# Twelve weight tiles of a split-precision gated MLP, each started at its own offset within 128 bytes

## The chip, the cores and the metric

The kernel runs on one NeuronCore of one Trainium2 chip. The metric is device time in microseconds of one execution. The time before is the median of 3 runs; one further execution was profiled.

## What is computed

The reference takes a transposed-channel attention over q, k, v (6016 rows of 256 channels) and sends its result through two gated feed-forward layers of width 1536:

```python
qn = q / (norm(q, axis=rows) + 1e-6);  kn = the same of k
a = softmax(kn^T @ qn / tau);  x = v @ a
def moe(x):                              # layer 1
    xn = x / sqrt(mean(x*x) + 1e-6) * rms_g
    g = xn @ w1_gate
    return (g * sigmoid(g) * (xn @ w1_val)) @ w1_out
def moe2(x):                             # layer 2
    return (sigmoid(x @ w2_gate) * (x @ w2_val)) @ w2_out
out = moe2(moe(x))
```

## The kernel before

All matrix products of the layers are made in the matmul format fp32r from operands that are split in a high and a low part: a product is hi x hi + hi x lo + lo x hi, three matmuls of 128x128 weights and up to 512 moving columns that add up in one PSUM bank (`three`, L682 to L684, and in `down`, L813 to L815). Activations are held transposed, channels on partitions, in blocks of 512 tokens: eleven full blocks (the trace's 128x512 matmuls) and a last one of 384.

For each block and layer TensorE walks over twelve slices j of 128 hidden channels. `up` makes gate and value of a slice (two banks, six matmuls each, weights from `w_hi_g`, `w_lo_g`, `w_hi_v`, `w_lo_v`, moving operands `xs` or `x2`, high and low). `down`, two slices behind, multiplies the gated slice (`h_hi`, `h_lo`) by the output weights (`w_hi_o`, `w_lo_o`) into two banks, three matmuls each. That makes 18 large matmuls per slice. The order of work is written out by hand: `plan` interleaves layer 2 of block b with layer 1 of block b+2, and every engine walks the same plan with semaphores between them. ScalarE makes the sigmoid and rounds to the high parts (L405, L411), VectorE multiplies and makes the low parts (L613, L617, L622). Into layer 2's slices `next_x` puts the next block of the attention product (`make_x`), its row sums of squares (`sum_squares`, L708, short fp32 matmuls with one moving column) and the spreading of the row factors (`spread_rms`, L717).

There are six weights: gate, value and out of layer 1 (g1, v1, o1) and of layer 2 (g2, v2, o2). Each has a tile `w_hi` and a tile `w_lo`, so twelve in all, of 3072 floats per partition (12288 bytes, 96 times 128). The raw fp32 weights (`w_raw`) are loaded by DMA on SP's queue to where `w_lo` will stand and are split in place: ScalarE rounds (L335, for o2 L331), VectorE (L463, layer 1) or GpSimd (L319, L315, layer 2) subtracts. The SBUF allocator puts the tiles one after another; a tile of 24 floats called `align` stands between the small tiles and the matmuls' activations. All twelve weight tiles and all moving tiles (`xs`, `x2`, `h_hi`, `h_lo`) begin at a multiple of 128 bytes.

Ahead of the layers TensorE multiplies q and k over 47 row tiles in plain fp32 (L751, two matmuls in the trace for each of the program), and then, while the softmax is made by the other engines, it runs products that nobody reads, to stay busy: `keep_warm` (L728). Fifty of them take `w_hi_g` of layer 1 both as weights and as moving operand. They differ in form. The first 23 are four plain ones, four with 126 weight columns, four with 96, four whose weight columns are 16 bytes apart, four whose 256 moving columns are 8 bytes apart, and three whose weights begin 4 bytes further on. Then follow six with 256 moving columns (before `sum_squares(0)`), four whose weights begin 8 bytes on and six whose weights begin 256 bytes on (before `spread_rms(0)`), and eleven more, six of which change between two PSUM banks and five of which take one weight column 128 times.

Of the kernel before, what the change touches and what calls it, by code (L numbers as in the profile page):

```python
# [23 lines left out]
F32 = mybir.dt.float32  # L24
F32R = mybir.dt.float32r
# [4 lines left out]
P = 128  # L30
SQ = 32
# [6 lines left out]

def build(nc, q, k, v, tau, rms_g, w1_gate, w1_val, w1_out, w2_gate, w2_val, w2_out, out):
    _, N, C = q.shape  # L40
    F = w1_gate.shape[1]
    CC = C // P
    J = F // P
    JG = J // GROUPS
# [48 lines left out]
    with ExitStack() as ctx:  # L93
        def sb(name, shape, dt=F32):
            return ctx.enter_context(nc.sbuf_tensor(name, shape, dt))
# [5 lines left out]
        W = ("g1", "v1", "o1", "g2", "v2", "o2")  # L101
        shape = {w: [P, J, C] if w[0] == "o" else [P, CC, F] for w in W}

        w_hi = {w: sb(f"w_hi_{w}", shape[w], F32R) for w in W[:3]}
        with ExitStack() as early:
            w_raw = {w: early.enter_context(nc.sbuf_tensor(f"w_raw_{w}", shape[w], F32)) for w in W}
        w_lo = {w: sb(f"w_lo_{w}", shape[w], F32R) for w in W[:3]}
        with ExitStack() as early:  # L110
            qk = early.enter_context(nc.sbuf_tensor("qk", [P, QK_SLOTS, 2, QK_TILES * C], F32))
            sq_qk = early.enter_context(nc.sbuf_tensor("sq_qk", [P, 2, 2, QK_TILES * C], F32))
            sum_sq = early.enter_context(nc.sbuf_tensor("sum_sq", [P, 2, 2 * C], F32))
        w_lo.update({w: sb(f"w_lo_{w}", shape[w], F32R) for w in W[3:]})
        w_hi.update({w: sb(f"w_hi_{w}", shape[w], F32R) for w in W[3:]})

        ident = sb("ident", [P, P])
        ones = sb("ones", [P, P])
# [21 lines left out]
        ps = ctx.enter_context(nc.psum_tensor("ps", [P, 8, BLOCK], F32))  # L140
        GATE, VALUE = (0, 2), (1, 3)
        Y, X = (4, 5), (6, 7)
# [530 lines left out]
        def _(pe):  # L673
# [13 lines left out]
            def make_x(b, vt):  # L687
                w = width(b)
                pe.wait_ge(vt_lo_done, b * 2 + 2)
                for d in range(CC):  # L690
                    three(ps[:, X[d], 0:w],
                          [(a_hi[:, c, d * P:(d + 1) * P], a_lo[:, c, d * P:(d + 1) * P], vt[0][:, c, 0:w],
                            vt[1][:, c, 0:w]) for c in range(CC)]).then_inc(x_made, 1)

            def sum_squares(b):
                nt = width(b) // P


                first = isinstance(b, int) and b == 0
                chunks_left = CC if first else 1  # L700
                if first:
                    pe.wait_ge(x_squared, CC)
                    pe.wait_ge(xg_done, 1)
                else:
                    pe.wait_ge(squares_added, b)
                for n in range(nt):
                    for c in range(chunks_left):
                        mm = nc.tensor.matmul(ps[:, X[0], n:n + 1], sq[:, c, n * P:(n + 1) * P], ones[:, 0:1],  # L708
                                              start=(c == 0), stop=(c == chunks_left - 1))
                mm.then_inc(ms_made, 1)  # L710

            def spread_rms(b, diag):

                w = width(b)
                for part in range(2):
                    pe.wait_ge(diag_done, b * 2 + part + 1)
                    mm = nc.tensor.matmul(ps[:, X[1], 0:w], ones_r[:, :], diag[part][:, 0, 0:w],  # L717
                                          start=(part == 0), stop=(part == 1))
                mm.then_inc(rinv_spread, 1)

            def keep_warm(n, weights, cols=None, bank=Y[1]):

                cols = w_hi["g1"][:, 0, 0:JG * P] if cols is None else cols
                dst = ps[:, bank, 0:JG * P]
                if cols.shape[1] < JG * P:
                    dst = ps[:, bank, 0:cols.shape[1]]
                for _ in range(n):
                    nc.tensor.matmul(dst[0:weights.shape[-1], :], weights, cols, start=True, stop=True)  # L728

            def column_norms():  # L730

# [12 lines left out]
            for i, slot, t0, n in chunks:  # L744
# [4 lines left out]
                for t in range(n):  # L749
                    for c in range(CC):  # L750
                        mm = nc.tensor.matmul(ps[:, RAW[c], 0:C], alternate(qk[:, slot, 1, t * C:(t + 1) * C], c),  # L751
                                              qk[:, slot, 0, t * C:(t + 1) * C],
                                              start=(t0 + t == 0), stop=(t0 + t == TILES - 1))
# [2 lines left out]
            nc.tensor.matmul(ps[:, SPREAD, 0:C], ones[:, :], q_diag.rearrange("p c m -> p (c m)"),  # L756
                             start=True, stop=True).then_inc(q_spread, 1)
            pe.wait_ge(w_hi_done, 1)
            any_w = w_hi["g1"]
            keep_warm(4, any_w[:, 0, 0:P])  # L760
            keep_warm(4, any_w[:, 0, 0:P - 2])
            keep_warm(4, any_w[:, 0, 0:96])
            keep_warm(4, any_w[:, 0, 0:JG * P:JG])
            keep_warm(4, any_w[:, 0, 0:P], any_w[:, 0, 0:JG * P:2])
            keep_warm(3, any_w[:, 0, 1:P + 1])
            pe.wait_ge(a_lo_done, CC)
            make_x(0, xs)
            keep_warm(6, any_w[:, 0, 0:P], any_w[:, 0, 0:JG * P // 2])
            sum_squares(0)
            pe.wait_ge(ones_r_done, 1)  # L770
            keep_warm(4, any_w[:, 0, 2:P + 2])
            keep_warm(6, any_w[:, 0, 64:P + 64])
            spread_rms(0, xs)
            for _ in range(3):
                keep_warm(1, any_w[:, 0, 0:P], bank=Y[0])
                keep_warm(1, any_w[:, 0, 0:P], bank=Y[1])
            keep_warm(5, any_w[:, 0, 0:1].broadcast_to([P, P]))

            def up(layer, b, j, x, parts_of_x):

# [122 lines left out]
```

## Time and profile before

| | |
|---|---|
| median of 3 runs | 1273.71 us (1273.67 to 1273.84) |
| the profiled execution | 1273.06 us, span of its instructions 1271.3 us |
| TensorE matmul busy | 1259.9 us, 99% of the span, 5710 matmuls |
| weight loads busy | 1059.0 us (83%) |
| VectorE, ScalarE, GpSimd busy | 659.7, 454.7 and 41.4 us |
| DMA X

A matmul's end is modelled and matmuls overlap in the array: one is printed as 0.39 us long although the next begins 0.23 us after it. What a matmul costs is the distance between two starts. The weight loads (PEld) run beside the matmul before.

### The profile page before, as it was taken

To read this page: it belongs to the slowest core of one execution; us is meant where nothing else is said; L and a number is where in the kernel's file an instruction comes from. 1 tells how busy PE (TensorE), PEld (TensorE's weight loads), DVE (VectorE), ACT (ScalarE), POOL (GpSimd) and SP (SyncE) were. 2 spreads that over 40 slices of the span, in tenths; PEclk is the share of its full clock that TensorE was granted. 3 is DMA by queue.
4 is the path that set the end of the run, shared out by engine and by line. 5 is a ranking of instruction groups with operands and counts; after the bars stand their busy time and mean duration, and the time that the engine had idled before them with its cause. 6 is when DMAs were issued, how large, how long until landed. Compare 5 with 4: busy or idle time off the path is not lost.

```text
span 1271.3 us, 15532 instructions
## 1 busy us (share of the span) xinstructions
PE 1259.9 (99%) x5710; PEld 1059.0 (83%) x5710; DVE 659.7 (52%) x1014; ACT 454.7 (36%) x737; POOL 41.4 (3%) x35
## 2 busy tenths in 40 slices
PE   8999999999999999999999999999999999999998
PEld 7878888888888888888888888888888888889888
DVE  6776654544554554554454455455455455446343
ACT  5453633333333333333333333333333333333332
POOL 0000600000000000000000000000000000000000
PEclk9999999999999999999999999999999999999999
DMA  9920000100100100010010010010010001000000
GB/s 345 305 87 1 1 1 1 34 0 0 33 0 0 33 0 0 8 25 0 0 33 0 0 33 0 0 33 0 0 29 4 0 0 29 1 1 18 1 17 13
DMA packets 60569, 34.43 MB, mean 27 GB/s; under 512 B 50816, under 2 KB 54144, under 8 KB 60544
## 3 DMA queue, kind: packets, MB, share of 16 engines
q1 hardware_dynamic: 60544, 34.09, 9.3%
q8 instruction: 16, 0.26, 0.1%
q14 instruction: 9, 0.07, 0.0%
HBM read 27.92 MB, written 6.16 MB: 27 GB/s over the span
## 4 chain that ended last, share of the span: by engine, by line
PE 98%; DMA 0%; DVE 0%; SPq 0%; POOL 0%; issue 0%; DVEq 0%
PE ps L682 21%; PE ps L684 21%; PE ps L683 21%; PE ps L813 10%; PE ps L815 10%; PE ps L814 10%; PE ps L751 3%; PE ps L708 1%; PE ps L728 1%; DMA qk<-in_k 0%; PE ps L717 0%; SPq L257 0%; POOL small L303 0%; PE ps L737 0%; DVE w_lo_v L463 0%
## 5 line engine op out<-in xcount | busy, mean ns | idle before, releaser
L617 DVE TENSOR_TENSOR h<-ps,h 128x512 f32<-128x512 f32 (+1 forms) x288 | 196.0, 680 | 304.9 <-PE ps L684 291.4
L411 ACT ACTIVATE h_hi<-h 128x512 fp32r<-128x512 f32 (+1 forms) x288 | 179.4, 623 | 397.8 <-DVE h L617 396.2
L405 ACT ACTIVATE h<-ps 128x512 f32<-128x512 f32 (+1 forms) x288 | 169.6, 589 | 376.6 <-PE ps L684 376.5
L622 DVE TENSOR_TENSOR h_lo<-h,h_hi 128x512 fp32r<-128x512 f32 (+1 forms) x288 | 199.3, 692 | 130.7 <-ACT h_hi L411 127.0
L815 PE MATMUL ps<-h_hi,w_lo_o 128*128 128x512 f32 (+1 forms) x576 | 221.6, 385 | 0.0
L813 PE MATMUL ps<-h_hi,w_hi_o 128*128 128x512 f32 (+1 forms) x576 | 221.5, 385 | 0.0
L814 PE MATMUL ps<-h_lo,w_hi_o 128*128 128x512 f32 (+1 forms) x576 | 221.5, 385 | 0.0
L613 DVE TENSOR_TENSOR h<-ps,h 128x512 f32<-128x512 f32 (+1 forms) x144 | 97.9, 680 | 148.6 <-ACT h L405 148.6
L815 PEld LDWEIGHTS ps<-h_hi,w_lo_o 128*128 128x128 f32 x576 | 108.1, 188 | 20.7
L813 PEld LDWEIGHTS ps<-h_hi,w_hi_o 128*128 128x128 f32 x576 | 108.1, 188 | 20.6
L814 PEld LDWEIGHTS ps<-h_lo,w_hi_o 128*128 128x128 f32 x576 | 108.1, 188 | 20.5
L682 PE MATMUL ps<-xs_hi,w_hi_g 128*128 128x512 f32 (+1 forms) x312 | 119.0, 381 | 0.6 <-DVE w_lo_v L463 0.6
L684 PE MATMUL ps<-xs_hi,w_lo_g 128*128 128x512 f32 (+1 forms) x312 | 118.8, 381 | 0.0
L683 PE MATMUL ps<-xs_lo,w_hi_g 128*128 128x512 f32 (+1 forms) x312 | 118.8, 381 | 0.0
L684 PE MATMUL ps<-xs_hi,w_lo_v 128*128 128x512 f32 (+1 forms) x312 | 118.7, 381 | 0.0
L682 PE MATMUL ps<-xs_hi,w_hi_v 128*128 128x512 f32 (+1 forms) x312 | 118.7, 381 | 0.0
L683 PE MATMUL ps<-xs_lo,w_hi_v 128*128 128x512 f32 (+1 forms) x312 | 118.7, 381 | 0.0
L682 PE MATMUL ps<-x_hi,w_hi_g 128*128 128x512 f32 x264 | 103.7, 393 | 0.0
L684 PE MATMUL ps<-x_hi,w_lo_g 128*128 128x512 f32 x264 | 102.9, 390 | 0.0
L682 PE MATMUL ps<-x_hi,w_hi_v 128*128 128x512 f32 x264 | 102.8, 389 | 0.0
L683 PE MATMUL ps<-x_lo,w_hi_g 128*128 128x512 f32 x264 | 102.8, 389 | 0.0
L684 PE MATMUL ps<-x_hi,w_lo_v 128*128 128x512 f32 x264 | 102.8, 389 | 0.0
(113 smaller groups left out, 1324.1 us busy)
## 6 DMA issues: line engine op xcount, KB each, us to landing
v_in<-in_v SPq DMA_DIRECT2D x44, 128.0 KB, 3.0
out<-out_sb SPq DMA_DIRECT2D x44, 128.0 KB, 2.4
qk<-in_q SPq DMA_DIRECT2D x10, 512.0 KB, 7.6
qk<-in_k SPq DMA_DIRECT2D x10, 512.0 KB, 9.1
w_raw_g<-in_moe_w_gate SPq DMA_DIRECT2D x6, 512.0 KB, 7.6
w_raw_v<-in_moe_w_val SPq DMA_DIRECT2D x6, 512.0 KB, 8.2
w_raw_o<-in_moe_w_out SPq DMA_DIRECT2D x6, 512.0 KB, 8.8
qk<-in_q SPq DMA_DIRECT2D x3, 256.0 KB, 3.3
```

The lines of the kernel that those rows point to most:

```text
L405: nc.scalar.activation(h[:, slot, 0:w], ps[:, GATE[slot], 0:w], ACT.Sigmoid).then_inc(sig_done, 1)
L411: nc.scalar.activation(h_hi[:, part, 0:w], h[:, slot, 0:w], ACT.Copy).then_inc(hi_done, 1)
L613: nc.vector.tensor_tensor(h[:, slot, 0:w], ps[:, GATE[slot], 0:w], h[:, slot, 0:w], ALU.mult).then_inc(gated_done, 1)
L617: nc.vector.tensor_tensor(h[:, slot, 0:w], ps[:, VALUE[slot], 0:w], h[:, slot, 0:w], ALU.mult).then_inc(h_done, 1)
L622: nc.vector.tensor_tensor(h_lo[:, part, 0:w], h[:, slot, 0:w], h_hi[:, part, 0:w].bitcast(F32), ALU.subtract).then_inc(lo_done, 1)
L682: nc.tensor.matmul(dst, s_hi, m_hi, start=(n == 0), stop=False)
L683: nc.tensor.matmul(dst, s_hi, m_lo, start=False, stop=False)
L684: mm = nc.tensor.matmul(dst, s_lo, m_hi, start=False, stop=(n == last))
L751: mm = nc.tensor.matmul(ps[:, RAW[c], 0:C], alternate(qk[:, slot, 1, t * C:(t + 1) * C], c), qk[:, slot, 0, t * C:(t + 1) * C], start=(t0 ...
L813: nc.tensor.matmul(dst, hi, h_hi[:, part, 0:w], start=(j == 0), stop=False)
L814: nc.tensor.matmul(dst, hi, h_lo[:, part, 0:w], start=False, stop=False)
L815: mm = nc.tensor.matmul(dst, lo, h_hi[:, part, 0:w], start=False, stop=(j == J - 1))
```

## The change

Every weight tile is allocated 32 floats longer (12416 bytes, 97 times 128), so that the tiles still begin at multiples of 128 bytes, and the 3072 floats that are used begin at an offset of their own in it. In bytes: high parts g1 16, v1 32, o1 48, g2 4, v2 120, o2 96; low parts g1 64, v1 80, o1 112, g2 8, v2 124, o2 0. The raw weights, which share the place of the low parts, have their offsets. The moving tiles still begin at multiples of 128 bytes, each 1536 bytes higher in SBUF. The second part of the change makes all matmuls of `keep_warm` alike: plain weights, 512 moving columns, one bank, 23 + 6 + 10 + 12 of them.

```diff
-        w_hi = {w: sb(f"w_hi_{w}", shape[w], F32R) for w in W[:3]}
+        START_HI = {"g1": 4, "v1": 8, "o1": 12, "g2": 1, "v2": 30, "o2": 24}
+        START_LO = {"g1": 16, "v1": 20, "o1": 28, "g2": 2, "v2": 31, "o2": 0}
+
+        def weight_tile(stack, name, w, dt, start):
+
+            tile = stack.enter_context(nc.sbuf_tensor(name, [P, CC * F + SQ], dt))
+            return tile[:, start:start + CC * F].rearrange("p (a b) -> p a b", a=shape[w][1])
+
+        w_hi = {w: weight_tile(ctx, f"w_hi_{w}", w, F32R, START_HI[w]) for w in W[:3]}
         with ExitStack() as early:
-            w_raw = {w: early.enter_context(nc.sbuf_tensor(f"w_raw_{w}", shape[w], F32)) for w in W}
-        w_lo = {w: sb(f"w_lo_{w}", shape[w], F32R) for w in W[:3]}
+            w_raw = {w: weight_tile(early, f"w_raw_{w}", w, F32, START_LO[w]) for w in W}
+        w_lo = {w: weight_tile(ctx, f"w_lo_{w}", w, F32R, START_LO[w]) for w in W[:3]}
...
-        w_lo.update({w: sb(f"w_lo_{w}", shape[w], F32R) for w in W[3:]})
-        w_hi.update({w: sb(f"w_hi_{w}", shape[w], F32R) for w in W[3:]})
+        w_lo.update({w: weight_tile(ctx, f"w_lo_{w}", w, F32R, START_LO[w]) for w in W[3:]})
+        w_hi.update({w: weight_tile(ctx, f"w_hi_{w}", w, F32R, START_HI[w]) for w in W[3:]})
...
-            keep_warm(4, any_w[:, 0, 0:P])
-            keep_warm(4, any_w[:, 0, 0:P - 2])
-            keep_warm(4, any_w[:, 0, 0:96])
-            keep_warm(4, any_w[:, 0, 0:JG * P:JG])
-            keep_warm(4, any_w[:, 0, 0:P], any_w[:, 0, 0:JG * P:2])
-            keep_warm(3, any_w[:, 0, 1:P + 1])
+            keep_warm(23)
             pe.wait_ge(a_lo_done, CC)
             make_x(0, xs)
-            keep_warm(6, any_w[:, 0, 0:P], any_w[:, 0, 0:JG * P // 2])
+            keep_warm(6)
             sum_squares(0)
             pe.wait_ge(ones_r_done, 1)
-            keep_warm(4, any_w[:, 0, 2:P + 2])
-            keep_warm(6, any_w[:, 0, 64:P + 64])
+            keep_warm(10)
             spread_rms(0, xs)
-            for _ in range(3):
-                keep_warm(1, any_w[:, 0, 0:P], bank=Y[0])
-                keep_warm(1, any_w[:, 0, 0:P], bank=Y[1])
-            keep_warm(5, any_w[:, 0, 0:1].broadcast_to([P, P]))
+            keep_warm(12)
```

No other instruction of any engine is added, removed or moved. On TensorE, from the last matmul of the first `make_x` to the first of the layers, this stood before:

```order
L684 MATMUL ps<-xs_hi,a_lo 128x512
L728 MATMUL ps<-w_hi_g 128x256 x6
L708 MATMUL ps<-ones,scratch 128x1 x8
L728 MATMUL ps<-w_hi_g 128x512 x10
L717 MATMUL ps<-xs_hi,ones_r 128x512
L717 MATMUL ps<-xs_lo,ones_r 128x512
L728 MATMUL ps<-w_hi_g 128x512 x11
L682 MATMUL ps<-xs_hi,w_hi_g 128x512
```

And this stands there now:

```order
L692 MATMUL ps<-xs_hi,a_lo 128x512
L732 MATMUL ps<-w_hi_g 128x512 x6
L716 MATMUL ps<-ones,scratch 128x1 x8
L732 MATMUL ps<-w_hi_g 128x512 x10
L725 MATMUL ps<-xs_hi,ones_r 128x512
L725 MATMUL ps<-xs_lo,ones_r 128x512
L732 MATMUL ps<-w_hi_g 128x512 x12
L690 MATMUL ps<-xs_hi,w_hi_g 128x512
```

Six matmuls ahead of the sums of squares are twice as wide, and one more stands ahead of the layers.

## Rows read from the trace of the kernel before

**Rows 1.** The page: busy time by engine, and the TensorE clock in 40 slices.
```profile
PE 1259.9 (99%) x5710; PEld 1059.0 (83%) x5710; DVE 659.7 (52%) x1014; ACT 454.7 (36%) x737; POOL 41.4 (3%) x35
PEclk9999999999999999999999999999999999999999
```

**Rows 2.** Chain of waits, stretch of one loop turn (start us, us, what).
```profile
497.14 0.79 PE ps L708 x8
...
599.19 0.79 PE ps L708 x8
```

**Rows 3.** Matmuls and loads by line and form (count, busy us, mean ns, idle us).
```profile
L815 PE MATMUL ps<-h_hi,w_lo_o 128*128 128x512 f32 x528 | 205.5, 389 | 0.0
L682 PE MATMUL ps<-x_hi,w_hi_g 128*128 128x512 f32 x264 | 103.7, 393 | 0.0
L683 PE MATMUL ps<-xs_lo,w_hi_v 128*128 128x512 f32 x264 | 102.7, 389 | 0.0
L813 PE MATMUL ps<-h_hi,w_hi_o 128*128 128x384 f32 x48 | 16.1, 336 | 0.0
L813 PEld LDWEIGHTS ps<-h_hi,w_hi_o 128*128 128x128 f32 x576 | 108.1, 188 | 20.6
```

**Rows 4.** Timeline of TensorE around the short matmuls of a loop turn.
```profile
599.03 0.95 PE L708 MATMUL ps<-ones,scratch 128*128 128x1 f32 x8
599.84 0.49 PE L682 MATMUL ps<-x_hi,w_hi_g 128*128 128x512 f32 x1
600.16 0.40 PE L683 MATMUL ps<-x_lo,w_hi_g 128*128 128x512 f32 x1
...
602.02 0.39 PE L682 MATMUL ps<-x_hi,w_hi_v 128*128 128x512 f32 x1
...
605.87 0.39 PE L684 MATMUL ps<-x_hi,w_lo_v 128*128 128x512 f32 x1
```

**Rows 5.** Timeline of TensorE, end of the q and k product, first `keep_warm` stage.
```profile
48.73 0.81 PE L751 MATMUL ps<-qk 128*128 128x256 f32 x3
49.38 0.59 PE L756 MATMUL ps<-scratch,ones 128*128 128x256 f32 x2
...
50.28 0.40 PE L728 MATMUL ps<-w_hi_g 128*128 128x512 f32 x1
...
53.07 0.63 PE L728 MATMUL ps<-w_hi_g 128*128 128x512 f32 x2
```

**Rows 6.** The same: weights 4 bytes on (54.68), then 8 bytes on (60.57 to 61.34).
```profile
54.68 0.63 PE L728 MATMUL ps<-w_hi_g 128*128 128x512 f32 x2
54.91 0.40 PE L728 MATMUL ps<-w_hi_g 128*128 128x512 f32 x1
...
60.88 0.62 PE L728 MATMUL ps<-w_hi_g 128*128 128x512 f32 x2
...
61.57 0.62 PE L728 MATMUL ps<-w_hi_g 128*128 128x512 f32 x2
```

**Rows 7.** Timeline of TensorE from `make_x(0)` to the layers.
```profile
57.91 0.87 PE L728 MATMUL ps<-w_hi_g 128*128 128x256 f32 x6
58.77 1.95 PE L708 MATMUL ps<-ones,scratch 128*128 128x1 f32 x16
60.57 2.54 PE L728 MATMUL ps<-w_hi_g 128*128 128x512 f32 x10
63.97 0.50 PE L717 MATMUL ps<-xs_hi,ones_r 128*128 128x512 f32 x1 [0.85 <-DVE xs_hi L530]
64.91 2.70 PE L728 MATMUL ps<-w_hi_g 128*128 128x512 f32 x11
67.45 0.39 PE L682 MATMUL ps<-xs_hi,w_hi_g 128*128 128x512 f32 x1
```

**Rows 8.** Timelines of ScalarE and VectorE in the same stretch.
```profile
58.11 0.60 ACT L359 ACTIVATE scratch<-ps 128x512 f32<-128x512 f32 x1 [0.78 <-PE ps L684]
...
66.49 1.29 DVE L545 TENSOR_TENSOR xs_lo<-x_raw,xs_hi 128x512 fp32r<-128x512 f32 x2
```

**Rows 9.** Timelines of ScalarE and VectorE: first weights split, and first use of the scores.
```profile
44.88 1.06 ACT L335 ACTIVATE w_hi_v<-w_raw_v 128x1024 fp32r<-128x1024 f32 x1 [0.16 <-DMA w_raw_v<-in_moe_w_val]
...
48.33 1.22 DVE L463 TENSOR_TENSOR w_lo_v<-w_raw_v,w_hi_v 128x1024 fp32r<-128x1024 f32 x1
50.51 0.48 DVE L574 SCALAR_TENSOR_TENSOR y<-ps,small,y 128x256 f32<-128x256 f32 x1 [0.96 <-ACT y L385]
```

**Rows 10.** The page, DMA issues (median us from issue to landing).
```profile
w_raw_g<-in_moe_w_gate SPq DMA_DIRECT2D x6, 512.0 KB, 7.6
```

More of the change, by code:

```diff
@@ L719, in spread_rms, with keep_warm @@
                 mm.then_inc(rinv_spread, 1)
[L721 to L726, printed above, removed]
+            def keep_warm(n):
                 for _ in range(n):
-                    nc.tensor.matmul(dst[0:weights.shape[-1], :], weights, cols, start=True, stop=True)
+                    nc.tensor.matmul(ps[:, Y[1], 0:JG * P], w_hi["g1"][:, 0, 0:P], w_hi["g1"][:, 0, 0:JG * P],
+                                     start=True, stop=True)
             def column_norms():
@@ L758, in _ @@
             pe.wait_ge(w_hi_done, 1)
-            any_w = w_hi["g1"]
-            keep_warm(4, any_w[:, 0, 0:P])
-            keep_warm(4, any_w[:, 0, 0:P - 2])
-            keep_warm(4, any_w[:, 0, 0:96])
-            keep_warm(4, any_w[:, 0, 0:JG * P:JG])
-            keep_warm(4, any_w[:, 0, 0:P], any_w[:, 0, 0:JG * P:2])
-            keep_warm(3, any_w[:, 0, 1:P + 1])
+            keep_warm(23)
             pe.wait_ge(a_lo_done, CC)
             make_x(0, xs)
-            keep_warm(6, any_w[:, 0, 0:P], any_w[:, 0, 0:JG * P // 2])
+            keep_warm(6)
             sum_squares(0)
             pe.wait_ge(ones_r_done, 1)
-            keep_warm(4, any_w[:, 0, 2:P + 2])
-            keep_warm(6, any_w[:, 0, 64:P + 64])
+            keep_warm(10)
             spread_rms(0, xs)
-            for _ in range(3):
-                keep_warm(1, any_w[:, 0, 0:P], bank=Y[0])
-                keep_warm(1, any_w[:, 0, 0:P], bank=Y[1])
-            keep_warm(5, any_w[:, 0, 0:1].broadcast_to([P, P]))
+            keep_warm(12)
             def up(layer, b, j, x, parts_of_x):
```

## The prediction

> **What bounds the kernel now.** I read the page first: matmuls are busy 99% of the span, every other engine at most 52%, and the granted clock is in the highest tenth in all 40 slices, so TensorE runs at its 2.4 GHz level and has nobody to wait for [rows 1]. The chain of waits says the same: one loop turn (layer 2 of a block, layer 1 of another) lasts 599.19 - 497.14 = 102.05 us, and every piece of it is TensorE's [rows 2]. A turn holds 24 slices of 18 large matmuls, 12 of the attention product and 2 of the spreading, 446 in all, beside 8 short ones of 0.79 us together. So a large matmul costs (102.05 - 0.79) / 446 = 0.2270 us. The groups by form say how many the weight tiles take part in: 15 groups like the first three lines of [rows 3], three of 528 and twelve of 264, 4752 matmuls with 512 columns, and 9 groups of 48 with 384 columns, 432: 5184 together. Any change of the distance between starts counts 5184 times: **1 ns is 5.2 us**, and the 2.5 us (0.2%) that a measurement here can tell from nothing is half a nanosecond.
>
> What to see in the timeline: the distance isn't one number. From 602.02 to 605.87 there are 17 steps, 0.2265 us each. But right behind the short matmuls, from 600.16 to 602.02, there are 8 steps in 1.86 us, 0.2325 each [rows 4]. So there is a settled distance of 0.2265 and an unsettled one of 0.2325, and TensorE needs about ten matmuls to settle. The plain fp32 matmuls of the q and k product, 256 columns twice through, are 0.65 / 3 = 0.217 apart [rows 5]; they begin at aligned places too. Something costs the fp32r matmuls some 10 ns each which those don't pay.
>
> **The change, term by term.**
>
> *Six wider filler matmuls ahead of the sums of squares.* Before, they begin at 57.91 and the sums at 58.77, just after ScalarE's squares end at 58.71: they are hidden [rows 7, 8]. With 512 columns they are 0.23 apart (60.88 to 61.57 has three in 0.69, [rows 6]), and the sums begin at 57.91 + 6 x 0.23 = 59.29, which is 0.52 us later. The cover (ScalarE's squares) is used up. What follows is a chain: sums, VectorE, GpSimd's power, VectorE's diagonal, then L717, before which TensorE idles 0.85 us [rows 7]. Filler in that idle time doesn't move it; the late sums do. **+0.52 us.**
>
> *Ten fillers before L717:* as many as before, hidden in front of the idle time. **0.** *The first 23:* twenty-three before and after, all some 0.23 apart whatever their form [rows 5]. **0.**
>
> *One more filler ahead of the layers (12 for 11).* The eleven run from 64.91 to 67.45; the first low part of x is ready about 67.14, halfway through the pair that begins at 66.49 and lasts 1.29 [rows 7, 8]. So the fillers end last and another one is on the path. **+0.23 us**, and no less, because the slack in front of it is negative already.
>
> *Splitting the weights at odd offsets.* The same instructions of the same sizes. The trace has no row of ScalarE or VectorE on a shifted tile; the bounds are 0 and one doubled instruction. The one nearest the path is L463 on `w_lo_v` (48.33, 1.22 us); behind it VectorE idles 0.96 us before L574 [rows 9]. Doubled, it gives 0.3 us. I take 0.
>
> *DMA to shifted places.* A load lands 7.6 us after its issue [rows 10]. The first value weights are on time by little (ScalarE waits 0.16 us for them), but their low part is made only at 48.33 while the high part is ready at 45.94, and then come the 0.96 us: 3.3 us of cover [rows 9]. Loads half as long again (3.8 us) would show 0.5 us, loads twice as long 4.3 us. I take 0, since 7.6 us is mostly queueing behind other loads; ends 0 and 4.3.
>
> *The weight loads and the matmuls themselves.* A load of 128 columns takes 188 ns in each of the groups [rows 3], of a distance of 227: 39 ns of cover. The question is whether matmul and load disturb each other by where they read. The rows nearest to it are the fillers with shifted weights: 4 bytes on, 0.23 (54.68 to 54.91); 8 bytes on, 0.69 / 3 = 0.230 [rows 6]. Plain aligned weights in the same unsettled state are 0.2325 apart [rows 4]. So shifted weights are no slower and no faster than aligned ones as far as three or four matmuls can show, and groups on tiles of different addresses have the same 389 ns and no idle time [rows 3]. **I take 0**; the ends are in the rivals.
>
> Here a rule of the Trainium skill meets the trace. The page "TensorE: Matmul & The Clock Gate", section "Part 2: What happens when you issue a matmul", says that TensorE has two independent SBUF read ports and that loading the next weights takes no read bandwidth from the running matmul. By it the offset is worth 0 and the kernel comes out at 1274.5. The same page's "Back-to-back issue gap" gives N/2.4 + 2.5 ns, 215.8 for 512 columns: the trace agrees for fp32 (217) and not for fp32r (226.5), so the rule isn't proof that nothing collides here.
>
> **The sum.** 0.52 + 0.23 = +0.75 us on the profiled execution: 1273.06 + 0.75 = 1273.81. The median of the runs stands 0.65 us above that execution: 1273.71 + 0.75 = **1274.5**. This case's own range, with the DMA and VectorE bounds, is 1273 to 1278.
>
> **The rivals.**
>
> *Slower: TensorE no longer settles.* The settled distance may exist only because every pair of operands begins at the same place in 128 bytes. In `up` the weight tile changes at hi to lo, lo to hi, and g to v: at four of six steps. If each change of offset disturbs like the short matmuls do, all 5184 run unsettled: (232.5 - 227.0) ns x 5184 = 28.5 us, **1303**. For it: the first filler stage, whose weight form changes every four, never settles: 50.28 to 53.07 is 12 steps in 2.79 us, 0.2325 each [rows 5], and that stage is 20 matmuls long, where ten suffice elsewhere. Against: its forms differ in more than the offset. If shifted weights settle, but at the 0.230 of the 8-byte fillers: 3.0 ns x 5184 = 15.6 us, 1290. It decides from the first disturbed 500 matmuls (2.5 us) on. Chance 0.28.
>
> *Slower: weights off a 16-byte boundary load longer.* Four tiles (both parts of g2 and v2) begin at 4, 8, 120 and 124 bytes. They serve the up matmuls of layer 2: six groups of 264, and 288 of the last block, 1872. If a shifted load reads a 33rd piece of 16 bytes where 32 took 188 ns, and TensorE waits for it, 5.9 ns x 1872 = 11 us, **1285**. Against: 39 ns of cover in every step. The Trainium skill's page "SBUF — State Buffer", section "Specifications (TRN2)", speaks of 16-byte lines and a penalty for each crossing to a new one; no run here shows that yet. Chance 0.08.
>
> *Faster: the extra 10 ns are collisions between weight load and moving operand that begin at the same place, and spreading the tiles removes them.* Then fp32r matmuls come down to the 0.2167 of the fp32 ones: 10.3 ns x 5184 = 53 us, 1221; half of it 1248. For it: the fp32 row, and that the distance can vary at all. Against: fillers at 4 and 8 bytes gain nothing visible. Chance 0.16.
>
> *The change doesn't do what it says.* The starts are counted in floats, four bytes each, and 97 x 128 bytes keep the tiles aligned, so the twelve offsets are real. This is no case of its own.
>
> **How the numbers follow.** No change 0.48, slower rivals 0.28 + 0.08, faster 0.16. The likeliest is no change: 1274.5. The range takes in its case with its bounds and both slower rivals, 1271 to 1304, and leaves out the faster case (0.16) and what is beyond 1304 (about 0.02). Within 0.2% (1271.2 to 1276.3): 0.48. Slower: 0.36. Faster: 0.16.
>
> **What would show it.** Right: 0.2265 in the middle of a loop turn, turns of 102.05 us, the sums of squares at 59.3, the layers from 68.2. The unsettled rival: 0.230 to 0.2325 in the middle of a turn and turns of 103.5 to 104.5 us, in layer 1 and layer 2 alike. The line rival: longer weight loads (194 ns) and a larger distance only in layer 2's up matmuls. The faster one: distances under 0.224. DMA: L463 on `w_lo_v` later than 49.3. What makes the forecast wrong is a distance that moves by more than half a nanosecond in the loop; nothing else in this change is large enough.

## The result and the profile after

| | before | after |
|---|---|---|
| median | 1273.78 us (4 runs) | 1296.03 us (4 runs, 1295.63 to 1296.72) |
| span of the profiled execution | 1271.3 us | 1294.3 us |
| one loop turn | 102.05 us | 104.00 us |

The change makes the kernel slower: ratio 1.0175, 95% interval [1.0158, 1.0193], 22.3 us. The forecast was 1274.5 us and no change, with a range to 1304 us. The time lies in the range only because the range took in the rival "TensorE no longer settles" (chance 0.28); the case that I held to be the likeliest (0.48) is not what happened.

The page after, busy time by engine and the clock row, answers to [rows 1]:

```profile
PE 1283.1 (99%) x5711; PEld 1061.4 (82%) x5711; DVE 657.3 (51%) x1014; ACT 454.8 (35%) x737; POOL 41.9 (3%) x35
PEclk9999999999999999999999999999999999999999
```

TensorE alone grew, by 23 us with one more matmul, and not by its clock: the granted clock is in the highest tenth in all 40 slices, as before. The chain of waits, one loop turn, answers to [rows 2]:

```profile
506.34 0.78 PE ps L716 x8
...
610.34 0.78 PE ps L716 x8
```

A turn is 104.00 us where it was 102.05. (104.00 - 0.78) / 446 = 0.2314 us for a large matmul, 4.4 ns more than 0.2270; times 5184 that is 22.8 us, the whole of the change. The groups by form (the same three as in [rows 3]) and the weight loads:

```profile
L810 PE MATMUL ps<-h_hi,w_lo_o 128*128 128x512 f32 x528 | 206.9, 392 | 0.0
L690 PE MATMUL ps<-x_hi,w_hi_g 128*128 128x512 f32 x264 | 104.5, 396 | 0.0
L691 PE MATMUL ps<-xs_lo,w_hi_v 128*128 128x512 f32 x264 | 103.5, 392 | 0.0
```
```profile
L808 PEld LDWEIGHTS ps<-h_hi,w_hi_o 128*128 128x128 f32 x576 | 108.2, 188 | 23.0
```

No matmul waits (idle 0.0), a load still takes 188 ns, and all three groups are longer than before (392, 396 and 392 ns for 389, 393 and 389), layer 1's (`xs`) as well as layer 2's (`x`). The timeline at the end of a turn, the last slice of layer 2 before the short matmuls, answers to [rows 4]:

```profile
606.02 0.39 PE L690 MATMUL ps<-x_hi,w_hi_g 128*128 128x512 f32 x1
...
610.18 0.95 PE L716 MATMUL ps<-ones,scratch 128*128 128x1 f32 x8
```

Eighteen steps in 4.16 us, 0.2311 each, 100 us after the last short matmuls; before, 0.2265 was reached within some ten matmuls of them. This is the picture that the prediction had given for the unsettled rival (turns of 103.5 to 104.5 us, both layers alike).

### The profile page after: what moved, and what is told of

Same layout as the page of the kernel before. It is cut to its first block, busy times and chain, and to the rows that moved or that the text cites. A ratio compares the mean times of both kernels' runs of the same rounds, so it can differ in the third digit from the quotient of the medians.

```text
span 1294.3 us, 15534 instructions
## 1 busy us (share of the span) xinstructions
PE 1283.1 (99%) x5711; PEld 1061.4 (82%) x5711; DVE 657.3 (51%) x1014; ACT 454.8 (35%) x737; POOL 41.9 (3%) x35
## 4 chain that ended last, share of the span: by engine, by line
PE 98%; DMA 1%; DVE 0%; SPq 0%; POOL 0%; issue 0%; DVEq 0%
PE ps L690 21%; PE ps L692 21%; PE ps L691 21%; PE ps L808 10%; PE ps L809 10%; PE ps L810 10%; PE ps L756 3%; PE ps L716 1%; PE ps L732 1%; DMA qk<-in_k 1%; PE ps L725 0%; SPq L265 0%; POOL small L311 0%; PE ps L742 0%; DVE w_lo_v L471 0%
## 5 line engine op out<-in xcount | busy, mean ns | idle before, releaser
L630 DVE TENSOR_TENSOR h_lo<-h,h_hi 128x512 fp32r<-128x512 f32 (+1 forms) x288 | 196.4, 682 | 130.7 <-ACT h_hi L419 127.1
L808 PE MATMUL ps<-h_hi,w_hi_o 128*128 128x512 f32 (+1 forms) x576 | 225.2, 391 | 0.0
L809 PE MATMUL ps<-h_lo,w_hi_o 128*128 128x512 f32 (+1 forms) x576 | 225.0, 391 | 0.0
L690 PE MATMUL ps<-xs_hi,w_hi_v 128*128 128x512 f32 (+1 forms) x312 | 121.5, 389 | 0.0
L692 PE MATMUL ps<-x_hi,w_lo_g 128*128 128x512 f32 x264 | 104.5, 396 | 0.0
L690 PE MATMUL ps<-x_hi,w_hi_g 128*128 128x512 f32 x264 | 104.5, 396 | 0.0
L691 PE MATMUL ps<-x_lo,w_hi_g 128*128 128x512 f32 x264 | 103.5, 392 | 0.0
```

The lines of the kernel that those rows point to most:

```text
L630: nc.vector.tensor_tensor(h_lo[:, part, 0:w], h[:, slot, 0:w], h_hi[:, part, 0:w].bitcast(F32), ALU.subtract).then_inc(lo_done, 1)
L690: nc.tensor.matmul(dst, s_hi, m_hi, start=(n == 0), stop=False)
L691: nc.tensor.matmul(dst, s_hi, m_lo, start=False, stop=False)
L692: mm = nc.tensor.matmul(dst, s_lo, m_hi, start=False, stop=(n == last))
L808: nc.tensor.matmul(dst, hi, h_hi[:, part, 0:w], start=(j == 0), stop=False)
L809: nc.tensor.matmul(dst, hi, h_lo[:, part, 0:w], start=False, stop=False)
```

## The experiments

I began with three theories. A: the offset of the weights from the moving operand sets the distance. B: it is the change of offset from one matmul to the next that disturbs. C: not the offsets but the longer tiles, the higher addresses or the fillers.

### All offsets back to 0

```diff
-        START_HI = {"g1": 4, "v1": 8, "o1": 12, "g2": 1, "v2": 30, "o2": 24}
-        START_LO = {"g1": 16, "v1": 20, "o1": 28, "g2": 2, "v2": 31, "o2": 0}
+        START_HI = {'g1': 0, 'v1': 0, 'o1': 0, 'g2': 0, 'v2': 0, 'o2': 0}
+        START_LO = {'g1': 0, 'v1': 0, 'o1': 0, 'g2': 0, 'v2': 0, 'o2': 0}
```

> The changed kernel with all twelve offsets put back to 0: tiles 12416 bytes long, moving tiles 1536 bytes higher, the new fillers. Theory A (the offset of the weights from the moving operand sets the distance between matmuls) and theory B (it is the change of offset from one matmul to the next that disturbs) both expect the time of before plus the fillers, 1274.5 us, and turns of 102.05 us. Theory C (the longer tiles or the higher addresses do it, not the offsets) expects 1296 us and turns of 104.0 us.

Measured: **1303.98 us**, ratio to before 1.0239 [1.0222, 1.0256]. The chain of waits of this kernel:

```profile
195.31 0.79 PE ps L716 x8
300.03 0.79 PE ps L716 x8
```

Turns of 104.72 us. A and B fall as I had put them: with no offset at all the kernel is slower than with the twelve. C didn't give the number either (1296). What is left of the change in this kernel is the tiles' length of 12416 bytes and the fillers. 12416 is 97 x 128: from one tile to the next the start moves on by 128 bytes within 256. Before, 12288 is 48 x 256, and all the matmuls' tiles began at the same place modulo 256. The moving tiles lie 1536 bytes higher, which is 6 x 256, so their place modulo 256 is the old one.

### All offsets 64 bytes, all offsets 4 bytes

```diff
+        START_HI = {'g1': 16, 'v1': 16, 'o1': 16, 'g2': 16, 'v2': 16, 'o2': 16}
+        START_LO = {'g1': 16, 'v1': 16, 'o1': 16, 'g2': 16, 'v2': 16, 'o2': 16}
```

The other kernel has 1 in the place of each 16 (the starts are counted in floats).

```diff
+        START_HI = {'g1': 1, 'v1': 1, 'o1': 1, 'g2': 1, 'v2': 1, 'o2': 1}
+        START_LO = {'g1': 1, 'v1': 1, 'o1': 1, 'g2': 1, 'v2': 1, 'o2': 1}
```

> All twelve tiles at the same offset, 64 bytes from the moving operands. Theory B expects no disturbance, since no matmul changes the offset: 1274.5 us. Theory A expects another time than 1274.5, in either direction, by up to 5 ns a matmul (26 us). Theory C expects 1296 us.

> All twelve tiles at the same offset, 4 bytes from the moving operands, so that each load of weights starts off a 16-byte boundary. Theory B expects 1274.5 us. Theory A expects a longer distance everywhere. The line theory (a load off a 16-byte boundary is longer) expects weight loads of 194 ns instead of 188 and more than 1274.5 us, where the kernel with 64 bytes stays at 1274.5.

Measured: **1298.8 us** (1.0200 [1.0183, 1.0217]) and **1301.12 us** (1.0218 [1.0201, 1.0235]). Both have the 128-byte steps in them, so they can't tell A from C by themselves. They do settle the line theory. Weight loads of the 4-byte kernel, by form:

```profile
L809 PEld LDWEIGHTS ps<-h_lo,w_hi_o 128*128 128x128 f32 x576 | 108.2, 188 | 23.8
```

188 ns and not 194: a load that begins off a 16-byte boundary isn't longer here.

### Fillers alone; 256 bytes of extra length; moving tiles 128 bytes on

Theory D took the place of the three: what counts is where weights and moving operand begin **modulo 256 bytes**.

The fillers alone:

```diff
-            keep_warm(6, any_w[:, 0, 0:P], any_w[:, 0, 0:JG * P // 2])
+            keep_warm(6)
...
+            keep_warm(12)
```

> The kernel before with the change's fillers alone (23 + 6 + 10 + 12 alike). All theories of the offsets expect +0.5 to +0.8 us (six wider fillers ahead of the sums of squares, one more ahead of the layers) and loop turns of 102.05 us. A theory that the fillers leave TensorE in another state for the layers expects more than 1290 us.

Measured: 1274.18 us, ratio 1.0003 [0.9994, 1.0012], and the same turns as before:

```profile
192.16 0.79 PE ps L708 x8
294.20 0.79 PE ps L708 x8
```

The kernel with offsets 0 and tiles 256 bytes longer:

```diff
-            tile = stack.enter_context(nc.sbuf_tensor(name, [P, CC * F + SQ], dt))
+            tile = stack.enter_context(nc.sbuf_tensor(name, [P, CC * F + 64], dt))
```

> The kernel with all offsets 0 and longer tiles, but the tiles 256 bytes longer and not 128, so that all twelve begin at the same place modulo 256 bytes (not modulo 512) as the moving tiles. Theory D (what counts is where weights and moving operand begin modulo 256 bytes) expects 1274.5 us and turns of 102.05 us. If the period is 512 bytes or more, about 1290 to 1304 us. If it is the longer tiles or the higher addresses as such, about 1304 us.

Measured: **1274.28 us** (ten runs, 1273.39 to 1276.24), ratio 1.0006 [0.9997, 1.0016]. The chain of waits:

```profile
192.32 0.79 PE ps L716 x8
294.37 0.79 PE ps L716 x8
```

Turns of 102.05 us. It has even longer tiles and higher addresses than the 1304 us kernel with offsets 0 and differs from it in 128 bytes per tile alone. So theory C falls, and the period isn't 512 bytes: the tiles' starts now differ by 256 bytes within 512, and that costs nothing.

The kernel before with the moving tiles 128 bytes on:

```diff
-        sb("align", [P, 24])
+        sb("align", [P, 56])
```

> The kernel before with the align tile 128 bytes longer: the weights lie where they lay, all moving tiles 128 bytes higher. Theory D expects the distance to leave 226.7 ns in every group (231 to 236), 1295 to 1310 us in all. If only the tiles' length mattered, 1273.7 us.

Measured in one run: **1301.22 us**, with one line of the kernel before changed. The chain of waits:

```profile
194.65 0.79 PE ps L708 x8
299.11 0.79 PE ps L708 x8
```

Turns of 104.46 us, as D had forecast: the twelve weight tiles lie where they lay, and only the moving tiles have moved against them.

### Sections of fillers at one offset each

```diff
-            keep_warm(4, any_w[:, 0, 0:P])
...
+            mv = any_w[:, 0, 0:JG * P]
...
+            for i in range(36):
+                s = 1
+                nc.tensor.matmul(ps[:, Y[i // 6 % 2], :], any_w[:, 0, s:s + P], mv, start=(i % 6 == 0), stop=(i % 6 == 5))
...
```

There is one such loop for each offset `s`, in floats.

> The kernel before with other fillers in the place of the first 23: for each of the offsets 4, 8, 16, 32, 48, 64, 80, 96, 112, 120 and 124 bytes a section of 36 matmuls on weights that begin there, then for each of them a section of 36 in which two matmuls on aligned weights are followed by one at the offset, as hi, hi, lo in the layers; 12 aligned ones behind each section. Theory A expects the steady distance in the first kind of section to differ by offset, 227 ns for 0 alone. Theory B expects 227 ns in all sections of the first kind and 230 to 234 in all of the second. Both parts of the computation's fillers are read by nobody. The time grows by some 240 us.

Chain of waits of this kernel (one run, 1516.55 us). L763 is on aligned weights, L766 4 bytes on, L772 8, L778 16, L784 32 and L826 124 bytes on, L820 120; L844 and L850 are of the second kind (two aligned, one at 16 or at 32 bytes).

```profile
49.99 5.47 PE ps L763 x24
55.47 8.37 PE ps L766 x36
...
66.59 8.30 PE ps L772 x36
...
77.64 8.16 PE ps L778 x36
...
88.53 8.39 PE ps L784 x36
...
155.34 8.16 PE ps L820 x36
...
166.22 8.34 PE ps L826 x36
...
199.51 8.16 PE ps L844 x36
...
210.39 8.39 PE ps L850 x36
```

36 matmuls in 8.16 us are 226.7 ns each, in 8.39 us 233.1. So a steady stream at a constant offset can stay unsettled for its whole section (A in a new form, and against B), and two offsets beside 0 settle, 16 and 120 bytes. The second kind settles at the same two offsets: a change of offset disturbs only where the offset itself does.

> The kernel before with other fillers in the place of the first 23: sections of 30 on weights that begin 16, 32, 48 ... 496 + 12 bytes further on (31 steps of 16 bytes), 12 aligned ones behind each; then sections with 384 moving columns in which the moving operand begins 128, 256, 384, 16 and 4 bytes on, with the weights left and with the weights moved by as much. Theory D: 226.7 ns at 256 bytes and at 16 and near 256 + 16, and not at 128 and 384. If the relation between the two operands counts and not the place of each, the sections that move both are at the aligned 173.3 ns. The fillers are read by nobody; the time grows by some 350 us.

In steps of 16 bytes, sections of 30 (one run, 1649.48 us). Chain of waits: 16, 32, 48 and 128, 144, 192, 240, 256, 272, 288, 304 and 400 bytes.

```profile
55.43 6.80 PE ps L763 x30
...
64.96 7.00 PE ps L767 x30
...
74.69 6.99 PE ps L771 x30
...
123.37 6.99 PE ps L791 x30
...
133.13 6.80 PE ps L795 x30
...
162.04 6.87 PE ps L807 x30
...
191.09 6.80 PE ps L819 x30
...
200.61 6.80 PE ps L823 x30
...
210.13 6.80 PE ps L827 x30
...
219.65 7.00 PE ps L831 x30
...
229.38 6.99 PE ps L835 x30
...
287.82 6.80 PE ps L859 x30
```

6.80 us are 226.7 ns, 7.00 us 233.3. It settles at 0, 16, 144 and 240 bytes, and 256 bytes further on every section is the same to 0.01 us: **the period is 256 bytes**. Then the sections with 384 moving columns, weights and moving operand shifted by: 0 and 128 bytes, 128 and 128, 16 and 16, 4 and 4.

```profile
358.44 5.28 PE ps L889 x30
...
365.81 5.20 PE ps L893 x30
...
409.66 5.26 PE ps L917 x30
...
424.29 5.40 PE ps L925 x30
```

5.20 us are 173.3 ns, the aligned value. Moved together by 128 bytes the pair settles, moved together by 16 or 4 bytes it doesn't. That the relation of the two starts alone counts is thus half right: the moving operand's own start counts too, below 128 bytes.

### The change's offsets without its 128-byte steps

The change with `CC * F + 64` for the tile's length, as above.

> The change's twelve offsets and fillers, with tiles 256 bytes longer in place of 128, so that the offsets are all that differs modulo 256 bytes. Theory D: the steady distances that the filler sections showed for these offsets, taken in the order hi, hi, lo, are 229.0 (g1), 233.0 (v1), 233.4 (o1), 231.7 (g2), 228.4 (v2) and 231.7 ns (o2), mean 231.2, so 4.5 ns over 226.7 and 23 us over the aligned kernel: 1297 us, give or take 5. If the 128 bytes of tile length made the whole slowdown of the change, 1274.5 us.

Measured: **1297.05 us** (four runs, 1296.76 to 1300.12), ratio 1.0187 [1.0170, 1.0204], turns of 104.13 us. So either part of the change alone is enough: offsets 23 us, 128-byte steps 30 us, both together 22 us. They don't add up. That fits with each only deciding whether the stream settles and at which unsettled mean. That the filler sections gave this time to a microsecond was luck in part: by the starts in the trace (200 to 1100 us) a step on v2's tiles took 232.3 ns for the 228.4 forecast, one on g1's 230.5 for 229.0 and one on v1's 231.8 for 233.0. Only the mean came out.

### All tiles at 16 bytes; high parts at 0 and low parts at 16

```diff
+        START_HI = {'g1': 4, 'v1': 4, 'o1': 4, 'g2': 4, 'v2': 4, 'o2': 4}
+        START_LO = {'g1': 4, 'v1': 4, 'o1': 4, 'g2': 4, 'v2': 4, 'o2': 4}
```

The other kernel has 0 for all in `START_HI` and the same `START_LO`. Both have tiles 256 bytes longer.

> All twelve tiles 16 bytes from the moving operands modulo 256 bytes. Theory D with the map of the filler sections: 16 is one of the places where the distance settles at 226.7 ns, so 1274.5 us and turns of 102.05 us. If only a common start modulo 256 settles in the layers, 1290 us or more.

> High parts at 0, low parts at 16 bytes from the moving operands modulo 256 bytes: two places that settle, changed at four of six steps. Theory D: 1274.5 us. What is left of theory B (each change of offset disturbs, though both places settle) expects 1290 to 1304 us.

Measured: **1301.17 us** (four runs, 1299.54 to 1302.15; 1.0213 [1.0196, 1.0230]) for all at 16, a miss, and **1274.46 us** in one run for 0 and 16 mixed, as theory D said. Chain of waits of the first, the short matmuls that open its first three turns:

```profile
91.34 0.79 PE ps L716 x8
...
193.68 0.79 PE ps L716 x8
...
298.31 0.79 PE ps L716 x8
```

The first turn took 102.34 us, the second 104.63, and so did all the later ones to 0.01 us. Timelines, a slice of the first turn and six steps of `up` in the third:

```profile
150.00 0.39 PE L690 MATMUL ps<-xs_hi,w_hi_g 128*128 128x512 f32 x1
...
152.72 0.39 PE L808 MATMUL ps<-h_hi,w_hi_o 128*128 128x512 f32 x1
```
```profile
303.24 0.40 PE L690 MATMUL ps<-x_hi,w_hi_g 128*128 128x512 f32 x1
...
304.64 0.40 PE L690 MATMUL ps<-x_hi,w_hi_v 128*128 128x512 f32 x1
```

Twelve steps in 2.72 us, 0.2267 each, in the first; 1.40 us for six, 233.3 ns each, in the second. So at 16 bytes both a settled and an unsettled rhythm last in one and the same kernel. The way in decides as far as these runs show it: the fillers at 16 bytes began out of a settled stream and stayed settled; in the layers the settled stretch of the first turn began behind the two spreading matmuls (L725 at 104.66, whose weights lie at 0) and ended with the short ones at 193.5. Why the spreading led into it only there is open, and so is whether the runs of 1299.5 and 1302.2 us had more or fewer settled turns. With 128 weight columns at 0 no lasting unsettled rhythm has been seen. And changing the offset at four of six steps costs nothing where high parts are at 0 and low parts at 16: theory B is finished.

### Shorter weight loads, and all other offsets

> The kernel before with other fillers in the place of the first 23: sections of 30 with 96, 64 and 32 weight columns, each on aligned weights and on weights 128 bytes further on; then 128 columns at 128 bytes; then sections of 24 at every offset from 4 to 252 bytes that is no multiple of 16; 12 aligned matmuls behind each. If what costs the 13.3 ns over 512 columns at 2.4 GHz is that the next weight load reads beside the moving operand, shorter loads make it smaller: with 32 weight columns 3 to 6 ns are left on aligned weights, and the shifted ones gain too. If it has nothing to do with the load, the distances stay at 226.7 and about 233 ns. The fillers are read by nobody; the time grows by some 450 us.

Chain of waits (one run, 1738.81 us): 96 weight columns aligned and at 128 bytes, 32 columns aligned and at 128 bytes, 128 columns at 128 bytes, then 128 columns at 12 bytes (L800) and at 20 (L804).

```profile
55.80 6.91 PE ps L764 x30
...
65.46 6.80 PE ps L768 x30
...
94.20 6.95 PE ps L780 x30
...
103.87 6.93 PE ps L784 x30
...
113.55 6.99 PE ps L788 x30
...
139.91 5.44 PE ps L800 x24
...
148.07 5.59 PE ps L804 x24
```

Nothing is under 226.7 ns, with a quarter of the weight columns either, although such a load is shorter in the trace (109 ns for 188). Thus the 13.3 ns over 512 columns at 2.4 GHz doesn't shrink with the load. But the load takes part in the rhythm: 96 columns settle at 128 bytes (6.80 us) and not on aligned weights (6.91), the other way round than 128 columns. Of the 48 offsets that are no multiple of 16, twelve settled in their section (12, 28, 36, 40, 100, 120, 132, 156, 216, 228, 244 and 252 bytes), at no regular distance. The others ran at 230 to 238 ns.

## Why the prediction was right and wrong

**What bounds the kernel: right.** TensorE's distance between starts times 5184 gave the price of everything: 4.4 ns give 22.8 us, and 22.3 were measured.

**The fillers, +0.75 us: right in place, too small to be measured.** The sums of squares began at 59.66 after and 58.77 before, 0.39 of it because the first q and k loads landed later in that execution (the q and k product begins at 9.83 instead of 9.44 in the chain): 0.50 for the 0.52 forecast. The fillers alone measured +0.43 us with an interval from -0.8 to +1.5.

**Splitting and DMA, 0: right as far as it shows.** Loads of w_raw_g landed in 7.0 us (7.6 before), and the layers began at 68.49 less 0.39, 68.1 for the 68.2 forecast.

**"I take 0" for loads and matmuls: this is the step that failed.** It rested on the fillers shifted by 4 and 8 bytes, three and four matmuls long, which were compared with aligned ones in the same unsettled state [rows 4, 6]. I had written that TensorE needs about ten matmuls to settle, so no stretch of three or four could show what decides the matter, whether it settles at all. With 36 in a row 4 bytes cost 232.5 ns and 8 bytes 230.6. The row that did bear on it, the first filler stage that stays at 0.2325 for 20 matmuls [rows 5], I gave to the rival and discounted.

**What I had overlooked** is that the change has two parts that count. I took "multiples of 128 bytes" for aligned and the longer tiles for neutral. The steps of 128 bytes alone cost 30 us. No row of the trace before could show it, since all tiles there are alike modulo 256 bytes; but that very fact should have widened the doubt, because the 0.2265 had been seen in one arrangement only.

**The unsettled rival** had the right mechanism, TensorE that doesn't settle, and a wrong reason: the change of offset at four of six steps. Its 1303 was worked out with 232.5 ns; the change ran at 231.4 and came to 1296, between that and the 1290 named beside it. That the range held is owed to this rival and not to the forecast. **The line rival** fell (188 ns). Its count was wrong too: the 288 matmuls of the last block are those of both layers, layer 2 has 144 of them, so 1728 and 10 us, not 1872 and 11. **The faster rival** fell: no offset, no shorter load and no mixture brought a steady fp32r stream under 226.7 ns. Nothing tried beats the kernel before; those that settle are equal to it.

**The two-port rule.** The Trainium skill's page "TensorE: Matmul & The Clock Gate", section "Part 2: What happens when you issue a matmul", says that loading the next weights takes no SBUF read bandwidth from the running matmul. It doesn't speak of placing; that the offset is worth 0 was my inference from it, and the runs disagree: 128 bytes make 27.5 us (the moving tiles 128 bytes on). The estimate of 215.8 ns for 512 columns, from N/2.4 + 2.5 in its section "Back-to-back issue gap", is by the page's words for an isolated matmul, and fp32r doesn't reach it in any arrangement tried (226.7 ns at best).

## What to carry to other kernels

When TensorE is the bound, lay all weight tiles and all moving tiles of fp32r matmuls at the same place modulo 256 bytes (a tile length that is a multiple of 256 bytes does it, 128 doesn't), and look at the distance between starts deep inside a long stream: about 227 ns at 512 columns is settled, 229 to 238 isn't. Judge a placement by sections of thirty matmuls or more, entered as the kernel enters them; three or four in a row, or a section that begins settled, say nothing safe, and at 16 bytes not even a turn that was settled for most of its length did. All this was measured with full 128x128 weights on one core; with fewer weight columns other places settle.

## What the runs showed that I had not expected

A steady fp32r stream costs 13.3 ns over its columns at 2.4 GHz at best (226.7 for 512, 173.3 for 384), and no less with shorter weight loads. Unsettled streams aren't noisy but run in fixed rhythms that repeat with the same mean for a whole section, often 233.3 ns (L767: 30 in 7.00 us) or 230.0 (L803: 6.90 us, at 176 bytes). The result is as regular in the layers: from the second turn on, the turns of 102.05, 104.00, 104.13, 104.46, 104.63 and 104.72 us repeat within 0.02 us in each kernel. What in the chip has a period of 256 bytes, and why some offsets hold two rhythms, stays open: it wasn't tried with moving operands of high and low parts placed differently, nor with other matmul formats.
